# Layer 1 of a fused attention and two-layer kernel on one core: sums of y in runs of 64, their place at a tile's edge, and three pairs by the plain product

## The chip, the cores and the metric

The kernel runs on one core of one Trainium2 chip. The metric is the device time of one execution in microseconds; the kernel before takes 1069.08 us (median of 3 runs, 1069.08 to 1069.72). Lower is better.

## The reference

q, k and v are 6016 x 256. Columns of q and k are normalised, a 256 x 256 softmax matrix is built from them, and v is multiplied by it. The result goes through two layers of the same form, x @ w_in (256 x 2048), an activation, @ w_out (2048 x 256). All is float32.

```python
def _attn_ref(q, k, v, tau):
    qn = q / (np.linalg.norm(q, axis=1, keepdims=True) + 1e-06)
    kn = k / (np.linalg.norm(k, axis=1, keepdims=True) + 1e-06)
    s = kn.transpose(0, 2, 1) @ qn / tau
    a = np.exp(s - s.max(-1, keepdims=True)); a /= a.sum(-1, keepdims=True) + 1e-09
    return v @ a
# layer 1 (moe):  h = x @ w_in;  g = where(h > 0, h, exp(min(h, 0)) - 1)   (ELU);   y = g @ w_out
# layer 2 (moe2): h = y @ w_in2; g = h / (1 + exp(-h))                     (SiLU);  out = g @ w_out2
```

## The kernel before

Every float32 operand of a big product is split into a high part (an fp32r copy, written by ScalarE) and a low part (what is left, written by VectorE); a product is three matmuls, high x high, high x low, low x high (PARTS).

Four stages follow each other: the softmax matrix (to about 45 us), its product with w_in (so that layer 1 works on v itself, to about 59 us), layer 1 (to about 595 us), layer 2. Layer 1 goes through 12 tiles of columns (512 columns each, the last two 448; `ONE`, a `Phase` each), layer 2 through 6 pairs of such tiles (`TWO`). The hidden 2048 units are 16 blocks of 128, worked on as 8 pairs. So a tile has 8 slots, k = 0 to 7, written out in `slot_one` of each engine; nothing but this order and the semaphores sets the times.

In slot k of a tile the engines do this:

- TensorE (PE): `up` for the two blocks of pair k (12 matmuls), then `one_down` for pair k - 2 (LAG_PAIRS). `up` of pair k waits for VectorE's `one_g` of pair k - 2, whose banks it overwrites (`u_g`); `one_down` waits for the low parts of its pair (`u_lo`).
- ScalarE (ACT): for each block `relu` (L744) and `exp` (L749), and between them the high part of the pair before (`normal_hi` L759; for a seven-product pair `one_plain_hi` L765 and L766, `one_sums_hi` L770), which waits for that pair's `one_g`.
- VectorE (DVE): `one_g` of pair k - 1 (L1015: ELU from ScalarE's exp and the banks; waits for the second exp), then that pair's low parts (`one_pair_parts`: `normal_lo` L1020, or for a seven-product pair `one_sums` L1031 to L1036, `one_plain_lo` L1043 and L1044, `one_sums_lo` L1049).

A pair goes down in one of two ways. `normal_down` is 12 matmuls of n columns. `wino_down` is a form of Strassen's product with seven products (21 matmuls of n/2 columns) that needs the extra sums above and leaves its results in other banks, from which `y_sums` and `y_rows` make y. `Phase.wino` says which pairs go that way: none in tile 0, pairs 0, 2, 4 in tiles 1 to 8, pairs 0, 2, 4, 6 in tiles 9 to 11.

At the tile's edge come: `one_copy` (ScalarE L778, COPY_LAG = 3 slots after the last seven-product pair), `y_sums` (VectorE L1067, L1069, L1071, SUM_LAG = 4 slots after it, which is slot 0 of the next tile, or slot 2 after tiles 9 and 10), `y_rows` (VectorE L1084 twice, slot 2 of the next tile, adds the banks of the normal pairs), `y1_hi_of` (ScalarE L791 twice, slot 3) and `y1_lo_of` (VectorE L1090 twice, slot 4), which write y's two parts for layer 2 in an order in which each run takes every fourth column. In slot 4 VectorE also turns v for the tile after (L939), in slot 6 it writes its low part (L945). In tiles 1 to 8 VectorE makes the forms of w_out2 (`form_sums` slot 0, `form_lo` slot 6). In tile 0 there is instead one piece of weights in each of slots 1 to 7: `weights_hi` (ScalarE L408) at the end of the slot, `weights_lo` (VectorE L414) at the end of the same slot. SyncE loads the pieces of w_in2 two at a time: the third waits for the low part of the first.

Layer 2's first tile (`TWO[0]`) begins while the last two pairs of layer 1 go down; its first `up` waits for the last exp of layer 1.

Of the kernel before, what the change touches and what calls it, by code (L numbers as in the profile page):

```python
# [34 lines left out]
F32 = mybir.dt.float32  # L35
# [4 lines left out]
P = 128  # L40
# [22 lines left out]
M7, M5, M6, M4, M1, M2, M3 = range(N_PRODUCTS)  # L63
ONE_PRODUCTS = (M1, M5, M7, M6, M2, M3, M4)
FIRST_OF_BANK = (M1, M7, M2, M4)
WINO_FEW, WINO_MORE = (0, 2, 4), (0, 2, 4, 6)
Y_U2, Y_U4, Y_P1, Y_U5, Y_U3, Y_P5 = range(6)
Y_SUMS = 5

# [16 lines left out]
def build(nc, q, k, v, tau, w_in1, w_out1, w_in2, w_out2, out):  # L86
# [19 lines left out]
    with ctx:  # L106
# [184 lines left out]
        class Phase:  # L291
# [3 lines left out]
            def __init__(self, tile, n, before):  # L295
                self.tile, self.n, self.before = tile, n, before
                self.x = xT[tile % 2]
                self.wino = () if tile == 0 else WINO_FEW if tile in FORM_PHASES else WINO_MORE
                self.wino_before = before.wino_before + len(before.wino) if before else 0
                self.v_next = None  # L300
                if tile != NT - 1:
                    self.v_next = (tile + 1, T_LAST if tile + 1 >= NT - 2 else T, xT[1 - tile % 2])
# [58 lines left out]

        def y_raw(ph, c):

            if ph.tile == 0:
                return y_banks[c][:, 0:ph.n]
            first = (Y_U4, Y_U5)[c] * ph.n // 2
            return ysum[:, first:first + ph.n]

        pair = lambda u, k: u.number * PAIRS + k

# [119 lines left out]
        def _(sp):  # L490
# [115 lines left out]
                        x_load(0, 0, a)  # L606


            sp.wait_ge(p1_down, NT * PAIRS - 1)
            ring_load(0, 0)  # L610
            ring_load(0, 1)
            sp.wait_ge(p1_down, NT * PAIRS)
# [54 lines left out]
        def _(act):  # L667
# [105 lines left out]
            def one_copy(ph):  # L773

                act.wait_ge(p1_down, one_pair(ph, ph.wino[-1]) + 1)
                if ph.tile >= 2:
                    act.wait_ge(y1_lo, CB * ph.tile)
                act.activation(y_sum(ph, slice(Y_P1, Y_P5 + 1, Y_P5 - Y_P1)),  # L778
                               bank[4][:, 0:ph.n].rearrange("p (s x) -> p s x", s=2), ACT.Copy).then_inc(m1_copy, 1)

            def y1_hi_of(ph):


                if ph.tile == 0:
                    act.wait_ge(w_split, n_split(IN2 + N_PIECES - 1))
                    act.wait_ge(p1_down, PAIRS)
                else:
                    act.wait_ge(d_spill, 16 * ph.tile)
                    act.wait_ge(c1_sum, Y_SUMS * ph.tile)
                for c in range(CB):  # L790
                    act.activation(y1T[:, 0, c, 0:ph.n].rearrange("p (m b) -> p m b", m=4),  # L791
                                   turned_back(y_raw(ph, c), 4), ACT.Copy).then_inc(y1_hi, 1)

            def one_forms_hi():
                act.wait_ge(f1_sum, 4)
# [82 lines left out]
            def tile(u):  # L878
                for k in range(PAIRS):
                    back = shifted(u, k, 1, PAIRS)  # L880
                    if u is TWO[0] and k == 0:
                        normal_hi(ONE[-1], PAIRS - 1)
                    if u is TWO[0] and k == 1:
                        one_copy(ONE[-1])
                    for i in range(4):
                        silu_first = u is TWO[0] and k == LAG_PAIRS
                        if silu_first:
                            silu(u, k, i)
                        if back:
# [26 lines left out]
        def _(dve):  # L916
# [143 lines left out]
            def y_sums(ph):  # L1060


                n = Y_SUMS * (ph.tile - 1)
                half = lambda b, i: bank[b][:, i * ph.n // 2:(i + 1) * ph.n // 2]
                dve.wait_ge(m1_copy, ph.tile)
                dve.wait_ge(p1_down, one_pair(ph, ph.wino[-1]) + 1)
                dve.tensor_tensor(y_sum(ph, Y_U2), half(*one_m[M6]), y_sum(ph, Y_P1), ALU.add).then_inc(c1_sum, 1)  # L1067
                dve.wait_ge(c1_sum, n + 1)
                dve.tensor_tensor(y_sum(ph, Y_U3), half(*one_m[M7]), y_sum(ph, Y_U2), ALU.add).then_inc(c1_sum, 1)  # L1069
                dve.wait_ge(c1_sum, n + 2)  # L1070
                dve.tensor_tensor(y_sum(ph, slice(Y_U4, Y_U5 + 1, 2)), y_sum(ph, slice(Y_U2, Y_U3 + 1, Y_U3 - Y_U2)),  # L1071
                                  y_sum(ph, slice(Y_P5, Y_P5 + 1)).broadcast_to([P, 2, ph.n // 2]),
                                  ALU.add).then_inc(c1_sum, 1)

            def y_rows(ph):

                n = Y_SUMS * (ph.tile - 1)
                dve.wait_ge(c1_sum, n + 3)
                for c in range(CB):
                    if c == 0:  # L1080
                        dve.wait_ge(y_done, ph.tile + 1)
                    else:
                        dve.wait_ge(p1_down, one_pair(ph, PAIRS - 1) + 1)
                    dve.tensor_tensor(y_raw(ph, c), y_banks[c][:, 0:ph.n], y_raw(ph, c), ALU.add).then_inc(c1_sum, 1)  # L1084

            def y1_lo_of(ph):
                for c in range(CB):
                    dve.wait_ge(y1_hi, CB * ph.tile + c + 1)
                    hi, lo = (y1T[:, x, c, 0:ph.n].rearrange("p (m b) -> p m b", m=4) for x in range(2))
                    dve.tensor_tensor(lo, turned_back(y_raw(ph, c), 4), hi.bitcast(F32),  # L1090
                                      ALU.subtract).then_inc(y1_lo, 1)

            def one_forms_sums():

# [44 lines left out]
            def slot_one(ph, k):  # L1139
                back = shifted(ph, k, 1, PAIRS)  # L1140
                if ph.tile == 1 and k == SLOT_ROWS:
                    y1_lo_of(ONE[0])
                if back:
                    one_g(*back)
                for tile in (ph, ph.before):
                    if tile and tile.wino and k + PAIRS * (tile is not ph) == tile.wino[-1] + SUM_LAG:
                        y_sums(tile)
                if ph.tile > 1 and k == SLOT_ROWS:
                    y_rows(ph.before)
                if back:  # L1150
                    one_pair_parts(*back)
                if ph.tile > 1 and k == SLOT_Y1_LO:
                    y1_lo_of(ph.before)
                if k == SLOT_V_TURN and ph.v_next:
                    v_transpose(*ph.v_next[:2])
                if k == SLOT_V_LO and ph.v_next:
                    vT_lo(*ph.v_next)
                if weights_in_slot(ph, k) is not None:
                    weights_lo(dve, weights_in_slot(ph, k))
                if ph.tile == 0 and k == SLOT_ONE_FORMS_SUM:  # L1160
                    one_forms_sums()
                if ph.tile == 0 and k == SLOT_ONE_FORMS_LO:
# [83 lines left out]
            def tile(u):  # L1246
                for k in range(PAIRS):
                    back = shifted(u, k, 1, PAIRS)
                    if u is TWO[0] and k == 0:
                        one_g(ONE[-1], PAIRS - 1)  # L1250
                        one_pair_parts(ONE[-1], PAIRS - 1)
                    if u is TWO[0] and k == 1:
                        y_sums(ONE[-1])
                    if back:
                        pair_sums(*back, 2)
# [52 lines left out]
        def _(pe):  # L1308
# [99 lines left out]
                elif ph.tile:  # L1408
                    pe.wait_ge(c1_sum, Y_SUMS * (ph.tile - 2) + 4 + c)

            def normal_down(ph, k):
                pe.wait_ge(u_lo, 2 * one_pair(ph, k) + 2)
                if k == 0:
                    pe.wait_ge(p_lo, CB * NWC)
                if ph.tile == 0:
                    pe.wait_ge(w_split, n_split(OUT1 + (2 * k + 1) * C // WP))
                for c in range(CB):
                    for n, (i, (x, y)) in enumerate((i, xy) for i in range(2) for xy in PARTS):
                        weights = wout1[:, 2 * k + i, x, c * P:(c + 1) * P]
                        g = by_turns(gpn[k % 2][:, y, i, 0:ph.n])  # L1420
                        last = k == PAIRS - 1 and n == 5
                        if ph.wino and k == 1 and c == 1 and n == 0:

                            for h in range(2):
                                pe.matmul(y_banks[c][:, h * ph.n // 2:(h + 1) * ph.n // 2], weights,
                                          g[:, h * ph.n // 4:(h + 1) * ph.n // 4, :], start=False, stop=False)
                        else:
                            mm = pe.matmul(y_banks[c][:, 0:ph.n], weights, g, start=k == 0 and n == 0, stop=last)  # L1428
                    if c == 0 and k == PAIRS - 1:
                        mm.then_inc(y_done, 1)  # L1430
                mm.then_inc(p1_down, 1)

            def wino_down(ph, k, first=0, end=N_PRODUCTS * len(PARTS)):

# [34 lines left out]
            def pair_up(u, k, i):  # L1469
# [7 lines left out]
                if u is TWO[0] and k < LAG_PAIRS:  # L1477
                    if k == 0 and i % 2 == 0:
                        pe.wait_ge(u_g, NT * PAIRS - 1 + i // 2)

                    pe.wait_ge(u_act, up_of(u, 0, 0) + H_FREE[4 * k + i])
                else:
                    pe.wait_ge(u_act, up_of(u, k, i))
                product(h_bank(u, k, i)[:, 0:u.n],
# [34 lines left out]
            def tile(u):  # L1519
                for k in range(PAIRS):  # L1520
                    back = shifted(u, k, LAG_PAIRS, PAIRS)
                    for i in range(4):
# [51 lines left out]
```

## Time and profile before

| | before |
|---|---|
| median of 3 runs | 1069.08 us (1069.08 to 1069.72) |
| the profiled execution | 1070.87 us |
| its span, first to last instruction | 1069.1 us |
| TensorE busy | 1023.8 us, 96% of the span |
| VectorE busy | 831.3 us, 78% |
| ScalarE busy | 722.0 us, 68% |
| mean granted TensorE clock | 0.986 |

Busy times are for the whole span, and matmuls are pipelined, so that a busy TensorE can still be fed late. What one step of the change is worth is read from the stage in which it lies.

### The profile page before, as it was taken

How to read it: one execution, taken by the hardware profiler on the slowest of the kernel's cores; microseconds unless marked ns; L12 is line 12 of the kernel's file. 1: busy time of each engine (PE TensorE's matmuls, PEld its weight loads, DVE VectorE, ACT ScalarE, POOL GpSimd, SP SyncE). 2: the span in 40 equal slices, each digit the busy share in tenths (PEclk: the TensorE clock that was granted, in tenths of full speed). 3: DMA queues.
4: the chain of work that ended last, by engine and by line, in shares of the span. 5: the costliest groups of instructions: out<-in, count | busy, mean ns of one | idle time of the engine just before them, and what ended most of it. 6: DMA issues, size and time to landing. Idle time of an engine off the chain costs nothing.

```text
span 1069.1 us, 14152 instructions
## 1 busy us (share of the span) xinstructions
PE 1023.8 (96%) x5085; PEld 904.8 (85%) x5085; DVE 831.3 (78%) x963; ACT 722.0 (68%) x1097; POOL 10.2 (1%) x11
## 2 busy tenths in 40 slices
PE   9997999999999899998999999999999999999998
PEld 8876787888888788887899878888888888888997
DVE  7767788878888787887878677787787787787786
ACT  6676667778667776777777665666666655666664
POOL 0300000000000000000000000000000000000000
PEclk9998999999999999999999999999999999999999
DMA  9902021221302213022030316425424434435333
GB/s 349 346 5 69 40 65 47 58 59 45 104 30 74 60 45 104 1 91 57 1 119 35 130 43 248 154 101 143 181 74 140 181 103 111 169 103 141 106 89 89
DMA packets 115066, 109.83 MB, mean 103 GB/s; under 512 B 89024, under 2 KB 97216, under 8 KB 112448
## 3 DMA queue, kind: packets, MB, share of 16 engines
q1 hardware_dynamic: 114400, 108.58, 31.7%
q8 instruction: 35, 0.57, 0.2%
q10 hardware_dynamic: 608, 0.49, 0.1%
q14 instruction: 23, 0.19, 0.1%
HBM read 83.23 MB, written 25.82 MB: 102 GB/s over the span
## 4 chain that ended last, share of the span: by engine, by line
PE 42%; DVE 23%; ACT 15%; issue 9%; DVEq 0%; ACTq 0%
PE banks L1314 22%; PE banks L1511 19%; ACT g_raw L749 6%; DVE g_raw L1015 5%; ACT g_raw L744 3%; DVE g_parts L1020 3%; ACT y1T_parts L791 2%; DVE g_raw_forms L1031 2%; ACT g_parts L759 2%; DVE y1T_parts L1090 2%; DVE g_form_parts L1043 2%; DVE g_raw_forms L1034 1%; DVE g_raw_forms L1036 1%; DVE v_transposed L939 1%; DVE g_form_parts L1044 1%
## 5 line engine op out<-in xcount | busy, mean ns | idle before, releaser
L1314 PE MATMUL banks<-xT_parts,a_w_in 128*128 128x512 f32 (+1 forms) x1152 | 271.3, 387 | 23.3 <-DVE g_raw L1015 23.2
L1314 PE MATMUL banks<-x_parts,w_in_parts 128*128 128x512 f32 (+1 forms) x1152 | 276.4, 376 | 4.7 <-ACT g_pair L850 2.6
L1314 PEld LDWEIGHTS banks<-xT_parts,a_w_in 128*128 128x128 f32 x1152 | 220.3, 195 | 56.9 <-DVE g_raw L1015 26.4
L1314 PEld LDWEIGHTS banks<-x_parts,w_in_parts 128*128 128x128 f32 x1152 | 215.9, 190 | 34.6 <-ACT g_pair L850 4.5
L1511 PE MATMUL banks<-g_pair_parts,w_forms 128*128 128x512 f32 (+1 forms) x987 | 239.3, 375 | 0.0
L1511 PEld LDWEIGHTS banks<-g_pair_parts,w_forms 128*128 128x128 f32 x987 | 186.5, 189 | 22.1
L850 ACT ACTIVATE g_pair<-banks 128x512 f32<-128x512 f32 (+1 forms) x192 | 112.9, 588 | 134.6 <-PE banks L1314 127.8
L1428 PE MATMUL banks<-g_parts,w_out_parts 128*128 128x512 f32 (+1 forms) x709 | 162.6, 376 | 0.0
L1428 PEld LDWEIGHTS banks<-g_parts,w_out_parts 128*128 128x128 f32 x709 | 133.7, 190 | 16.3
L1015 DVE SCALAR_TENSOR_TENSOR g_raw<-g_raw,banks 128x1024 f32<-128x1024 f32 (+1 forms) x96 | 114.5, 1193 | 25.0 <-ACT g_raw L749 25.0
L1197 DVE TENSOR_TENSOR g_pair_parts<-g_forms,g_pair_parts 128x1024 fp32r<-128x1024 f32 (+1 forms) x96 | 115.2, 1201 | 21.9 <-ACT g_pair_parts L859 21.8
L1020 DVE TENSOR_TENSOR g_parts<-g_raw,g_parts 128x1024 fp32r<-128x1024 f32 (+1 forms) x60 | 72.4, 1207 | 69.1 <-ACT g_parts L759 68.6
L859 ACT ACTIVATE g_pair_parts<-g_forms 128x1024 fp32r<-128x1024 f32 (+1 forms) x96 | 99.4, 1037 | 37.1 <-PE banks L1511 33.2
L749 ACT ACTIVATE g_raw<-g_raw 128x512 f32<-128x512 f32 (+1 forms) x192 | 118.1, 615 | 3.1
L744 ACT ACTIVATE g_raw<-banks 128x512 f32<-128x512 f32 (+1 forms) x192 | 110.0, 573 | 1.3 <-PE banks L1314 1.3
L1184 DVE TENSOR_TENSOR g_forms<-g_pair 128x1024 f32<-128x1024 f32 (+1 forms) x48 | 57.7, 1202 | 65.7 <-ACT g_pair L850 65.6
L759 ACT ACTIVATE g_parts<-g_raw 128x1024 fp32r<-128x1024 f32 (+1 forms) x60 | 62.6, 1043 | 56.0 <-issue 47.8
L1203 DVE TENSOR_TENSOR g_pair_parts<-g_pair,g_pair_parts 128x1536 fp32r<-128x1536 f32 (+1 forms) x48 | 82.5, 1719 | 3.5 <-ACT g_pair_parts L866 3.5
L866 ACT ACTIVATE g_pair_parts<-g_pair 128x1024 fp32r<-128x1024 f32 (+1 forms) x96 | 78.8, 822 | 0.6 <-PE banks L1511 0.6
L765 ACT ACTIVATE g_form_parts<-g_raw 128x512 fp32r<-128x512 f32 (+1 forms) x36 | 22.4, 622 | 78.5 <-DVE g_raw L1015 78.5
L1452 PE MATMUL banks<-g_form_parts,w_out_parts 128*128 128x256 f32 (+1 forms) x324 | 56.9, 285 | 10.7 <-DVE g_form_parts L1049 5.6
L1452 PEld LDWEIGHTS banks<-g_form_parts,w_out_parts 128*128 128x128 f32 x324 | 47.5, 195 | 19.0 <-DVE g_form_parts L1049 10.3
(112 smaller groups left out, 855.2 us busy)
## 6 DMA issues: line engine op xcount, KB each, us to landing
w_forms<-w_forms SPq DMA_DIRECT2D x48, 896.0 KB, 4.7
y_parts<-y1T_parts SPq DMA_DIRECT2D x10, 1024.0 KB, 4.1
x_parts<-y_parts SPq DMA_DIRECT2D x10, 1024.0 KB, 7.0
w_forms<-w_out_forms SPq DMA_DIRECT2D x8, 896.0 KB, 4.2
early_qk<-q SPq DMA_DIRECT2D x23, 256.0 KB, 7.7
early_qk<-k SPq DMA_DIRECT2D x22, 256.0 KB, 8.0
out<-out_tile SPq DMA_DIRECT2D x40, 128.0 KB, 2.7
v_in<-v SPq DMA_DIRECT2D x36, 128.0 KB, 3.6
```

Source lines behind the costliest of these rows:

```text
L744: act.activation(raw_units(ph, k)[:, i, :], h_ps[f % 4][:, 0:ph.n], ACT.Relu, scale=-1.0).then_inc(u_relu, 1)
L749: act.activation(e, e, ACT.Exp, scale=-1.0).then_inc(u_act, 1)
L759: act.activation(gpn[k % 2][:, 0, :, 0:ph.n], raw_units(ph, k), ACT.Copy).then_inc(u_hi, 2)
L850: act.activation(g2[:, k % 2, i, 0:u.n], h_bank(u, k, i)[:, 0:u.n], ACT.Silu).then_inc(u_act, 1)
L859: act.activation(gp2[k % 2][:, 0, 3 + 2 * s:5 + 2 * s, 0:u.n], t_sb[:, 2 * s:2 * s + 2, 0:u.n], ACT.Copy).then_inc(t_hi, 1)
L1015: dve.scalar_tensor_tensor(g, g, -1.0, two_banks[k % 2][:, :, 0:ph.n], ALU.add, ALU.max).then_inc(u_g, 1)
L1020: dve.tensor_tensor(part(1), raw_units(ph, k), part(0).bitcast(F32), ALU.subtract).then_inc(u_lo, 2)
L1197: dve.tensor_tensor(part(1), t_sb[:, 2 * s:2 * s + 2, 0:u.n], part(0).bitcast(F32), ALU.subtract).then_inc(t_lo, 1)
L1314: mm = pe.matmul(dst, lhsT, rhs, start=first and n == 0, stop=last and n == len(todo) - 1)
L1428: mm = pe.matmul(y_banks[c][:, 0:ph.n], weights, g, start=k == 0 and n == 0, stop=last)
L1452: mm = pe.matmul(bank[b][:, half * ph.n // 2:(half + 1) * ph.n // 2], weights, by_turns(gpw[:, y, operand, 0:ph.n // 2]), start=k == 0 and ...
L1511: mm = pe.matmul(m_banks[m][:, 0:u.n], ring[k % N_RING][:, form, x, :], by_turns(gp2[k % 2][:, y, operand, 0:u.n]), start=k == 0 and part ...
```

## The change

- `y_sum`'s slots hold each half of a tile as four runs of 64 (of 56 in a short tile) in place of plain order. The reading by every fourth column moves from `y1_hi_of` and `y1_lo_of`, which read SBUF, to `one_copy`, `y_sums` and `y_rows`, which read the banks.
- `Phase.wino` is (0, 2, 4) in every tile but tile 0. So pair 6 of tiles 9, 10, 11 is a normal pair; `one_copy` of these tiles comes in slot 7, `y_sums` in slot 0 of what follows.
- VectorE's slot: `y_rows` comes ahead of `one_g`; `y_sums` comes behind `one_pair_parts`.
- `weights_lo` of a piece comes one slot after its `weights_hi`.
- At the layer boundary the first four `up` of layer 2 no longer wait for the last exp of layer 1; a normal pair goes down in four shares between them; SyncE's wait ahead of the first two loads of the ring is for an earlier pair.

```diff
-WINO_FEW, WINO_MORE = (0, 2, 4), (0, 2, 4, 6)
+ONE_WINO = (0, 2, 4)
-                self.wino = () if tile == 0 else WINO_FEW if tile in FORM_PHASES else WINO_MORE
+                self.wino = ONE_WINO if tile else ()
         def y_raw(ph, c):
-            if ph.tile == 0:
-                return y_banks[c][:, 0:ph.n]
             first = (Y_U4, Y_U5)[c] * ph.n // 2
-            return ysum[:, first:first + ph.n]
+            return ysum[:, first:first + ph.n].rearrange("p (h m b) -> p h m b", h=2, m=4)
+        half_turned = lambda x: x.rearrange("p (b m) -> p m b", m=4)
+        half_plain = lambda x: x.rearrange("p (m b) -> p m b", m=4)
+        def y_and_part(ph, c, x):
+            part = y1T[:, x, c, 0:ph.n]
             if ph.tile == 0:
+                return turned_back(y_banks[c][:, 0:ph.n], 4), part.rearrange("p (m b) -> p m b", m=4)
+            return y_raw(ph, c).rearrange("p h m b -> p m h b"), part.rearrange("p (m h b) -> p m h b", m=4, h=2)
...
-            sp.wait_ge(p1_down, NT * PAIRS - 1)
+            sp.wait_ge(p1_down, one_pair(ONE[-1], ONE[-1].wino[-1]) + 1)
...
-                dve.tensor_tensor(y_sum(ph, Y_U2), half(*one_m[M6]), y_sum(ph, Y_P1), ALU.add).then_inc(c1_sum, 1)
+                dve.tensor_tensor(half_plain(y_sum(ph, Y_U2)), half_turned(half(*one_m[M6])),
+                                  half_plain(y_sum(ph, Y_P1)), ALU.add).then_inc(c1_sum, 1)
...
-                    dve.tensor_tensor(y_raw(ph, c), y_banks[c][:, 0:ph.n], y_raw(ph, c), ALU.add).then_inc(c1_sum, 1)
+                    dve.tensor_tensor(y_raw(ph, c), y_banks[c][:, 0:ph.n].rearrange("p (h b m) -> p h m b", h=2, m=4),
+                                      y_raw(ph, c), ALU.add).then_inc(c1_sum, 1)
...
             def slot_one(ph, k):          # VectorE
                 back = shifted(ph, k, 1, PAIRS)
+                if ph.tile > 1 and k == SLOT_ROWS:
+                    y_rows(ph.before)
                 if back:
                     one_g(*back)
+                    one_pair_parts(*back)
                 for tile in (ph, ph.before):
                     if tile and tile.wino and k + PAIRS * (tile is not ph) == tile.wino[-1] + SUM_LAG:
                         y_sums(tile)
-                if ph.tile > 1 and k == SLOT_ROWS:
-                    y_rows(ph.before)
-                if back:
-                    one_pair_parts(*back)
...
-                if weights_in_slot(ph, k) is not None:
-                    weights_lo(dve, weights_in_slot(ph, k))
+                if back and weights_in_slot(*back) is not None:
+                    weights_lo(dve, weights_in_slot(*back))
...
-                    pe.wait_ge(u_act, up_of(u, 0, 0) + H_FREE[4 * k + i])
+                if u is TWO[0] and k < LAG_PAIRS:
+                    if H_FREE[4 * k + i]:
+                        pe.wait_ge(u_act, up_of(u, 0, 0) + H_FREE[4 * k + i])
...
                         elif k == 0:
-                            wino_down(ONE[-1], PAIRS - 2, *PARTS_OF_SLOT[i:i + 2])
+                            normal_down(ONE[-1], PAIRS - 2, 3 * i, 3 * i + 3)
```

## Rows read from the trace of the kernel before

**Rows 1.** Waits of PE over the span: us in total, times, longest.

```profile
PE banks L1314 <- DVE g_raw L1015: 23.2, 14, 4.2
```

**Rows 2.** Stretches: length, busy (count) of PE, PEld, DVE, ACT, POOL, clock, DMA.

```profile
300.00:345.00 45.00, 41.60 (x221) 36.27 (x220) 36.57 (x48) 33.09 (x54) 0.00 (x0) 1.00 0.22 62
...
650.00:1053.00 403.00, 403.00 (x1908) 358.33 (x1907) 316.67 (x314) 250.54 (x354) 0.00 (x0) 1.00 0.42 132
```

**Rows 3.** PE in order of time, tile 4: start, length, line, idle before.

```profile
320.35 2.86 PE L1314 MATMUL banks<-xT_parts,a_w_in 128*128 128x512 f32 x12 [1.90 <-DVE g_raw L1015]
...
324.35 0.60 PE L1452 MATMUL banks<-g_form_parts,w_out_parts 128*128 128x256 f32 x3 [1.14 <-DVE g_form_parts L1049]
```

**Rows 4.** DVE in order of time, slot 4 of tile 4 to slot 2 of tile 5.

```profile
309.73 1.22 DVE L1015 SCALAR_TENSOR_TENSOR g_raw<-g_raw,banks 128x1024 f32<-128x1024 f32 x1 [0.44 <-ACT g_raw L749]
313.92 1.23 DVE L1020 TENSOR_TENSOR g_parts<-g_raw,g_parts 128x1024 fp32r<-128x1024 f32 x1 [2.97 <-ACT g_parts L759]
315.06 2.98 DVE L1090 TENSOR_TENSOR y1T_parts<-y_sums,y1T_parts 128x512 fp32r<-128x512 f32 x2
...
319.13 1.17 DVE L1015 SCALAR_TENSOR_TENSOR g_raw<-g_raw,banks 128x1024 f32<-128x1024 f32 x1
...
324.73 1.22 DVE L1015 SCALAR_TENSOR_TENSOR g_raw<-g_raw,banks 128x1024 f32<-128x1024 f32 x1 [0.44 <-ACT g_raw L749]
...
330.76 1.22 DVE L1015 SCALAR_TENSOR_TENSOR g_raw<-g_raw,banks 128x1024 f32<-128x1024 f32 x1
333.22 1.22 DVE L1020 TENSOR_TENSOR g_parts<-g_raw,g_parts 128x1024 fp32r<-128x1024 f32 x1 [1.25 <-ACT g_parts L759]
334.81 1.22 DVE L1015 SCALAR_TENSOR_TENSOR g_raw<-g_raw,banks 128x1024 f32<-128x1024 f32 x1 [0.37 <-ACT g_raw L749]
...
337.48 1.22 DVE L1020 TENSOR_TENSOR g_parts<-g_raw,g_parts 128x1024 fp32r<-128x1024 f32 x1
...
339.55 1.21 DVE L1015 SCALAR_TENSOR_TENSOR g_raw<-g_raw,banks 128x1024 f32<-128x1024 f32 x1
...
343.53 1.22 DVE L1049 TENSOR_TENSOR g_form_parts<-g_raw_forms,g_form_parts 128x1024 fp32r<-128x1024 f32 x1 [0.19 <-ACT g_form_parts L770]
345.20 1.22 DVE L1015 SCALAR_TENSOR_TENSOR g_raw<-g_raw,banks 128x1024 f32<-128x1024 f32 x1 [0.45 <-ACT g_raw L749]
346.34 1.28 DVE L1084 TENSOR_TENSOR y_sums<-banks,y_sums 128x512 f32<-128x512 f32 x2
```

**Rows 5.** ACT in order of time, from the end of slot 3 of tile 4.

```profile
309.60 2.78 ACT L791 ACTIVATE y1T_parts<-y_sums 128x512 fp32r<-128x512 f32 x2
```

**Rows 6.** Groups by line, shapes kept apart: busy us, mean ns, idle before.

```profile
L1090 DVE TENSOR_TENSOR y1T_parts<-y_sums,y1T_parts 128x512 fp32r<-128x512 f32 x18 | 25.9, 1481 | 0.0
...
L1090 DVE TENSOR_TENSOR y1T_parts<-banks,y1T_parts 128x512 fp32r<-128x512 f32 x2 | 1.3, 687 | 0.9 <-ACT y1T_parts L791 0.9
...
L945 DVE TENSOR_TENSOR xT_parts<-v_transposed,xT_parts 128x512 fp32r<-128x512 f32 x18 | 11.6, 684 | 0.0
...
L671 ACT ACTIVATE xT_parts<-v_transposed 128x512 fp32r<-128x512 f32 x18 | 10.2, 618 | 0.0
```

**Rows 7.** DVE in order of time, tile 0.

```profile
62.97 1.22 DVE L1015 SCALAR_TENSOR_TENSOR g_raw<-g_raw,banks 128x1024 f32<-128x1024 f32 x1 [2.41 <-ACT g_raw L749]
...
80.28 1.22 DVE L414 TENSOR_TENSOR w_out_parts<-early_w_out,w_out_parts 128x1024 fp32r<-128x1024 f32 x1 [1.31 <-ACT w_out_parts L408]
...
93.61 1.23 DVE L414 TENSOR_TENSOR w_in_parts<-weight_stage,w_in_parts 128x1024 fp32r<-128x1024 f32 x1 [2.35 <-ACT w_in_parts L408]
...
111.84 1.22 DVE L1015 SCALAR_TENSOR_TENSOR g_raw<-g_raw,banks 128x1024 f32<-128x1024 f32 x1
```

**Rows 8.** PE at the start of layer 2.

```profile
595.24 1.92 PE L1314 MATMUL banks<-x_parts,w_in_parts 128*128 128x512 f32 x6 [2.10 <-ACT g_raw L749]
...
611.96 0.81 PE L1511 MATMUL banks<-g_pair_parts,w_forms 128*128 128x512 f32 x3
...
626.72 1.56 PE L1314 MATMUL banks<-x_parts,w_in_parts 128*128 128x512 f32 x6 [1.65 <-ACT g_pair L850]
```

More of the change, by code:

```diff
@@ L362, in y_raw @@
         def y_raw(ph, c):
+            first = (Y_U4, Y_U5)[c] * ph.n // 2
+            return ysum[:, first:first + ph.n].rearrange("p (h m b) -> p h m b", h=2, m=4)
[3 more added lines that the diff above has]
+            part = y1T[:, x, c, 0:ph.n]
             if ph.tile == 0:
-                return y_banks[c][:, 0:ph.n]
-            first = (Y_U4, Y_U5)[c] * ph.n // 2
-            return ysum[:, first:first + ph.n]
+                return turned_back(y_banks[c][:, 0:ph.n], 4), part.rearrange("p (m b) -> p m b", m=4)
+            return y_raw(ph, c).rearrange("p h m b -> p m h b"), part.rearrange("p (m h b) -> p m h b", m=4, h=2)
         pair = lambda u, k: u.number * PAIRS + k
@@ L777, in one_copy @@
                     act.wait_ge(y1_lo, CB * ph.tile)
-                act.activation(y_sum(ph, slice(Y_P1, Y_P5 + 1, Y_P5 - Y_P1)),
-                               bank[4][:, 0:ph.n].rearrange("p (s x) -> p s x", s=2), ACT.Copy).then_inc(m1_copy, 1)
+                act.activation(y_sum(ph, slice(Y_P1, Y_P5 + 1, Y_P5 - Y_P1)).rearrange("p s (m b) -> p s m b", m=4),
+                               bank[4][:, 0:ph.n].rearrange("p (s b m) -> p s m b", s=2, m=4), ACT.Copy).then_inc(m1_copy, 1)
             def y1_hi_of(ph):
@@ L790, in y1_hi_of @@
                 for c in range(CB):
-                    act.activation(y1T[:, 0, c, 0:ph.n].rearrange("p (m b) -> p m b", m=4),
-                                   turned_back(y_raw(ph, c), 4), ACT.Copy).then_inc(y1_hi, 1)
+                    y, part = y_and_part(ph, c, 0)
+                    act.activation(part, y, ACT.Copy).then_inc(y1_hi, 1)
             def one_forms_hi():
@@ L882, in tile @@
                         normal_hi(ONE[-1], PAIRS - 1)
-                    if u is TWO[0] and k == 1:
-                        one_copy(ONE[-1])
                     for i in range(4):
@@ L1066, in y_sums @@
                 dve.wait_ge(p1_down, one_pair(ph, ph.wino[-1]) + 1)
-                dve.tensor_tensor(y_sum(ph, Y_U2), half(*one_m[M6]), y_sum(ph, Y_P1), ALU.add).then_inc(c1_sum, 1)
+                dve.tensor_tensor(half_plain(y_sum(ph, Y_U2)), half_turned(half(*one_m[M6])),
+                                  half_plain(y_sum(ph, Y_P1)), ALU.add).then_inc(c1_sum, 1)
                 dve.wait_ge(c1_sum, n + 1)
-                dve.tensor_tensor(y_sum(ph, Y_U3), half(*one_m[M7]), y_sum(ph, Y_U2), ALU.add).then_inc(c1_sum, 1)
+                dve.tensor_tensor(half_plain(y_sum(ph, Y_U3)), half_turned(half(*one_m[M7])),
+                                  half_plain(y_sum(ph, Y_U2)), ALU.add).then_inc(c1_sum, 1)
                 dve.wait_ge(c1_sum, n + 2)
@@ L1088, in y1_lo_of @@
                     dve.wait_ge(y1_hi, CB * ph.tile + c + 1)
-                    hi, lo = (y1T[:, x, c, 0:ph.n].rearrange("p (m b) -> p m b", m=4) for x in range(2))
-                    dve.tensor_tensor(lo, turned_back(y_raw(ph, c), 4), hi.bitcast(F32),
-                                      ALU.subtract).then_inc(y1_lo, 1)
+                    (y, hi), (_, lo) = (y_and_part(ph, c, x) for x in range(2))
+                    dve.tensor_tensor(lo, y, hi.bitcast(F32), ALU.subtract).then_inc(y1_lo, 1)
             def one_forms_sums():
@@ L1251, in tile @@
                         one_pair_parts(ONE[-1], PAIRS - 1)
-                    if u is TWO[0] and k == 1:
                         y_sums(ONE[-1])
@@ L1409, in rows_free, with normal_down @@
                     pe.wait_ge(c1_sum, Y_SUMS * (ph.tile - 2) + 4 + c)
-            def normal_down(ph, k):
-                pe.wait_ge(u_lo, 2 * one_pair(ph, k) + 2)
+            def normal_down(ph, k, first=0, end=2 * 2 * len(PARTS)):
+                if first == 0:
+                    pe.wait_ge(u_lo, 2 * one_pair(ph, k) + 2)
                 if k == 0:
@@ L1416, in normal_down @@
                     pe.wait_ge(w_split, n_split(OUT1 + (2 * k + 1) * C // WP))
[L1417 to L1429, printed above, removed]
+                for n in range(first, end):
+                    c, i, (x, y) = n // 6, n // 3 % 2, PARTS[n % 3]
+                    weights = wout1[:, 2 * k + i, x, c * P:(c + 1) * P]
+                    g = by_turns(gpn[k % 2][:, y, i, 0:ph.n])
+                    if ph.wino and k == 1 and n == 6:
+                        for h in range(2):
+                            pe.matmul(y_banks[c][:, h * ph.n // 2:(h + 1) * ph.n // 2], weights,
+                                      g[:, h * ph.n // 4:(h + 1) * ph.n // 4, :], start=False, stop=False)
+                    else:
+                        mm = pe.matmul(y_banks[c][:, 0:ph.n], weights, g, start=k == 0 and n % 6 == 0,
+                                       stop=k == PAIRS - 1 and n % 6 == 5)
+                    if n == 5 and k == PAIRS - 1:
                         mm.then_inc(y_done, 1)
-                mm.then_inc(p1_down, 1)
+                    if n == 11:
+                        mm.then_inc(p1_down, 1)
             def wino_down(ph, k, first=0, end=N_PRODUCTS * len(PARTS)):
```

## The prediction

> **What bounds the kernel now.** First the waits of PE: of the 45 us of the span in which it was not busy, 23.2 us went, in 14 waits of up to 4.2 us, to the ELU of layer 1 (`one_g`, L1015) [rows 1]. Then the stretches: layer 2, from 650 to 1053 us, has PE busy for all of its 403.00 us, so nothing that happens there can be hidden or regained and every microsecond won ahead of it reaches the end; a tile of layer 1 has PE busy for 41.60 of 45.00 us [rows 2]. Last the timeline of one tile. PE waits 1.90 us for an ELU and 1.14 us for low parts [rows 3], both on VectorE. The ELU of the same slot starts at 319.13, and PE's matmuls at 320.35 [rows 3, 4]. So layer 1 is not bound by PE. It is bound by a chain that goes to and fro between VectorE and ScalarE: ELU, its high part, the next exps, the next ELU. The reader is to read the starts of L1015 in rows 4 as the beat of that chain: 309.73, 319.13, 324.73, 330.76, 334.81, 339.55, 345.20, steps of 9.40, 5.60, 6.03, 4.05, 4.74 and 5.65 us. With the 4.07 us and the 5.66 us of slots 2 and 3, worked from the same timeline, they make a tile of 45.2 us. PE's own work in it is the floor: at most 41.8 us by its busy share [rows 2], and 40.8 by its matmuls, which follow each other at about 0.21 us per 512 columns (403.00 us over 1908 [rows 2]; closer, by the timeline, 16 `up` at 1.30, five normal pairs at 2.59, three of seven products at 2.34).
>
> **The change, part by part.**
>
> 1. *The order of y's sums.* Writing y's high part takes 2.78 us for two halves [rows 5], its low part 2.98 us [rows 4], 1481 ns each over 18 of them, against 684 ns (VectorE) and 618 ns (ScalarE) for the same 512 columns read from SBUF in runs of 32 [rows 6]. With runs of 64 I take these two values: ScalarE wins 1.6 us per tile and VectorE 1.6 us. Both lie on the chain, one behind the other: in that slot VectorE sits idle for 2.97 us until ScalarE, delayed by L791, has written the high part (313.92), then writes y's low part, turns v and only then comes to the ELU [rows 4]. Step 9.40 becomes 6.2 or less: -3.2 us. Is the reading by fours dear in its new place? The row nearest to it is y's low part of tile 0, which reads the banks by every fourth column and an SBUF operand: 687 ns [rows 6]; I take no cost. The other end is the SBUF price: 0.8 us more per 512 columns, in `y_rows` twice and in `y_sums` once, 2.4 us a tile on the chain.
>
> 2. *`y_sums` behind the low parts.* Now it fills the time in which VectorE waits for the high part: in the slot without it that gap is 1.25 us (333.22, 2.46 us after its ELU), in the slot with it L1020 follows at once (337.48, 2.67 us after) [rows 4]. It took 1.53 us (334.81 + 1.14 to 337.48). In the new order: 2.46 us to the low part, 1.14 for it (313.92 to 315.06), 1.53 for `y_sums`, 0.93 for the sums of w_out2's forms, 6.06 us in all instead of 4.74: +1.3 us. Behind the waiting low part `y_sums` itself now queues; PE needs it only in slot 2.
>
> 3. *`y_rows` ahead of the ELU.* The low parts of the pair before leave VectorE free at 343.53 + 1.14 = 344.67; the exps are ready at 345.20. Two `y_rows` take 1.2 us, to 345.87: the ELU is 0.7 us late [rows 4]. Its own wait, for the last normal pair, is over by then, as PE works two slots ahead of it. What it wins, some 0.4 us of PE in that slot, is off the chain.
>
>    Parts 1 to 3 on tiles 2 to 8: -3.2 + 1.3 + 0.7 = -1.2, and by the single rows of this tile (y's writes 1.65 instead of 1.6 us each) -1.3 us. Seven tiles: **-9 us**. A tile is then 43.9 us, still over PE's 40.8; PE is next late for the low parts of pairs 0 and 4, as now.
>
> 4. *Three pairs by the plain product.* The chain's step with a seven-product pair is 5.65 us (339.55 to 345.20), with a normal one 4.05 [rows 4]: -1.6 us for tile 9, 1.4 for each short one (x 448/512). PE gets 0.25 us more in tile 9 and nothing in the short ones; it has that room. With it `y_sums` comes away from slot 2, where it stood between two ELUs in tiles 10 and 11 (-1 us each) and goes to slot 0. Tile 9: -3.2 (y), -1.6, +1.1 (part 2 without forms), +0.7: -3.1. Tiles 10 and 11: -2.7 each, the same at 7/8. Together **-8.5 us**.
>
> 5. *`weights_lo` a slot later*, tile 0. Its ELUs go from 62.97 to 111.84 [rows 7] in seven steps, of 6.15 us but for two (9.71 and 8.41), since VectorE waits for the high part of the same slot's piece: 1.31 us in an ordinary slot, 2.35 us in the one in which ScalarE writes v's first [rows 7]. A slot later the piece is ready: steps of 2.46 + 1.14 + 1.14 = 4.74. Slot 1 (no piece any more) wins 2.1, slots 2 and 3 1.4 each, slot 4 0.25 (it turns v in that gap), slot 5 2.4, slot 6 0.2, slot 7 1.4: 9.2 us, less 1.14 for the last piece in slot 0 of tile 1. **-8 us**. PE (5.2 us a slot) keeps up but for short waits. On SyncE's queue the loads of the third and fourth piece of w_in2 go out a slot later relative to the work, and the load of the first forms behind them; these took 4.0 us to land in this stretch, and ScalarE wants them 6.3 and about 4 us after. The last has no room; it costs up to 0.5 us of ScalarE, beside the chain.
>
> 6. *The layer boundary.* PE idles 2.10 us until the last exp, and then runs at a granted clock of 0.90 over the next stretch: 16.72 us from 595.24 to 611.96 [rows 8] for matmuls that take 14.9 at full rate (8 `up` at 1.30, 24 of 448 columns at 0.189). Without the wait and the gap: -0.6 and -1.8. PE then waits 1.65 us for a SiLU [rows 8] that is behind y's high part on ScalarE (2.6 us there), and 0.75 us for one behind the low part; with these at half, -2.2. **-4.6 us**. The earlier ring loads win nothing; they had landed.
>
> Sum: -9 - 8.5 - 8 - 4.6 = -30 us. The profiled execution took 1070.87 us, 1.8 over its span and 1.8 over the median of 1069.08, so that it comes to 1040.7 and the median to **1039 us**.
>
> By the skill: the row shows 1481 ns for a reading of SBUF by every fourth float and 684 ns for runs [rows 6]. The Trainium skill (SBUF — State Buffer, the section on ports, its note on "cachelines") says that SBUF has lines of 16 bytes and that each access that crosses to a new line pays; the trace agrees. The same note gives PSUM lines of 8 bytes and a slowdown of matmuls for any non-contiguous access, which speaks against moving the stride there; for VectorE's reading the 687 ns row does not agree, and for a matmul's no run here shows it.
>
> **Rivals.**
>
> A. *The stride costs in the banks what it cost in SBUF.* 2.4 us on the chain for ten tiles: -30 + 24 = 1063 us. For it: the new instructions have a walk of four dimensions that no row has. Against: 687 ns. 8%. (This is what the PSUM rule named above would do here if it held for VectorE.)
>
> B. *y's writes are slow for another reason than the stride*, such as meeting PE's and the other engine's reads at that moment, and stay at 1.4 us. For it: the same two instructions took only 1.05 us each in tile 10, by its timeline. Then parts 2 and 3 stand alone: +2.0 us on seven tiles, +14, tiles 9 to 11 -2, boundary -2.4, tile 0 -8: +2 us, 1071; and with the loads of part 5 late, up to 1079. This is the slower case, and it decides from where a write of y keeps over 1.2 us. Against: tile 0's 687 ns. 6%.
>
> C. *PE becomes the bound again.* Its slack falls to 3 us a tile, in gaps of up to 1.4 us; where the granted clock falls to 1.2 GHz, as it did after 4.2 us of waiting in tile 0, a slot of 5.2 us takes up to 3 us more. If half of the ten tiles lose 2 us: 1049 us, range 1044 to 1056. 17%.
>
> D. *The change takes the chain below what I counted*, as gaps close that I left: 1031 us. 4%.
>
> **How the numbers follow.** The forecast, 1039 (1034 to 1044), has 65%; A 8, B 6, C 17, D 4. To hold 8 in 10 the range takes forecast and C: 1033 to 1056. A measurement of this kernel tells 0.2%, 2.1 us, from no change. Faster: all but B, less 0.01 for what I have not thought of, 0.93; B divided, 0.03 within and, with that 0.01, 0.04 slower.
>
> **What would show it.** L1090 and L791 on y_sums near 690 and 620 ns; L1084 and L1067 as before (683, 418); steps of L1015 at an edge of 6.1 and 6.3 us and of 6.1 in place of 9.4; ELUs of tile 0 ending near 103; layer 2's first matmul near 569; a tile of 43.9 us. Wrong: a tile of 45 us or more, L1084 over 1 us, or PE idle in layer 2's steady part.

## The result, and the profile after

The changed kernel takes 1039.74 us (median of 4 runs, 1038.93 to 1039.96) against 1069.08: ratio 0.9724, 95% interval 0.9707 to 0.9741. The forecast was 1039. The profiled execution took 1039.91 us, its span is 1038.1, 31.0 us less than before; VectorE is busy for 806.8 us and ScalarE for 702.1, some 25 and 20 less; the mean granted TensorE clock is 1.0.

One slip of names first: the stretch that the rows and the prediction call tiles 4 and 5 holds, counted from 0 as the kernel counts, tiles 5 and 6. No number depends on it.

The waits of PE in the kernel after, where [rows 1] stood, and the two stretches that answer to [rows 2] (columns as there):

```profile
PE banks L1460 <- DVE g_form_parts L1055: 17.1, 17, 1.1
PE banks L1320 <- DVE g_raw L1021: 2.8, 4, 1.5
```

```profile
285.00:328.00 43.00, 41.03 (x218) 35.42 (x217) 34.04 (x49) 31.59 (x54) 0.00 (x0) 1.00 0.23 64
625.00:1020.00 395.00, 395.00 (x1869) 351.13 (x1868) 311.12 (x309) 246.29 (x347) 0.00 (x0) 1.00 0.41 129
```

The waits for the ELU have gone from 23.2 to 2.8 us, and what is next late is what the prediction named, the low parts of seven-product pairs: 17.1 us in 17 waits, two in each of tiles 2 to 8 and one in tiles 1, 9 and 10. PE still does not bind layer 1, and layer 2 still has no idle time.

VectorE of the kernel after over one edge, for [rows 4]; L1021 is the ELU, L1026 the low part of a normal pair, L1099 y's low part, L1073 the first of `y_sums`, L1092 `y_rows`:

```profile
300.12 1.22 DVE L1021 SCALAR_TENSOR_TENSOR g_raw<-g_raw,banks 128x1024 f32<-128x1024 f32 x1 [0.44 <-ACT g_raw L757]
302.66 1.23 DVE L1026 TENSOR_TENSOR g_parts<-g_raw,g_parts 128x1024 fp32r<-128x1024 f32 x1 [1.32 <-ACT g_parts L767]
303.80 1.29 DVE L1099 TENSOR_TENSOR y1T_parts<-y_sums,y1T_parts 128x512 fp32r<-128x512 f32 x2
...
306.17 1.18 DVE L1021 SCALAR_TENSOR_TENSOR g_raw<-g_raw,banks 128x1024 f32<-128x1024 f32 x1
...
321.86 1.22 DVE L1021 SCALAR_TENSOR_TENSOR g_raw<-g_raw,banks 128x1024 f32<-128x1024 f32 x1 [0.36 <-ACT g_raw L757]
324.33 1.23 DVE L1026 TENSOR_TENSOR g_parts<-g_raw,g_parts 128x1024 fp32r<-128x1024 f32 x1 [1.24 <-ACT g_parts L767]
325.47 0.42 DVE L1073 TENSOR_TENSOR y_sums<-banks,y_sums 128x256 f32<-128x256 f32 x1
...
327.92 1.22 DVE L1021 SCALAR_TENSOR_TENSOR g_raw<-g_raw,banks 128x1024 f32<-128x1024 f32 x1
...
331.92 1.23 DVE L1055 TENSOR_TENSOR g_form_parts<-g_raw_forms,g_form_parts 128x1024 fp32r<-128x1024 f32 x1 [0.20 <-ACT g_form_parts L778]
333.06 1.28 DVE L1092 TENSOR_TENSOR y_sums<-banks,y_sums 128x512 f32<-128x512 f32 x2
334.26 1.21 DVE L1021 SCALAR_TENSOR_TENSOR g_raw<-g_raw,banks 128x1024 f32<-128x1024 f32 x1
```

The reader is to see three steps from ELU to ELU. 300.12 to 306.17 is 6.05 us where it was 9.40: the wait ahead of the low part is 1.32 us instead of 2.97, and y's low part takes 1.29 instead of 2.98. 321.86 to 327.92 is 6.06 where it was 4.74: VectorE idles 1.24 us ahead of L1026, and `y_sums` comes only behind it. 327.92 to 334.26 is 6.34 where it was 5.65: `y_rows` stands in front of an ELU that could have begun.

The groups that answer to [rows 6]:

```profile
L1099 DVE TENSOR_TENSOR y1T_parts<-y_sums,y1T_parts 128x512 fp32r<-128x512 f32 x18 | 11.6, 684 | 0.0
...
L1092 DVE TENSOR_TENSOR y_sums<-banks,y_sums 128x512 f32<-128x512 f32 x18 | 11.5, 682 | 0.0
...
L800 ACT ACTIVATE y1T_parts<-y_sums 128x512 fp32r<-128x512 f32 x18 | 10.2, 615 | 0.0
```

y's two writes are at the price of runs, and `y_rows`, which now reads the banks by fours, is as before (682 ns; it was 683 by the same view of before).

VectorE in tile 0, for [rows 7]; the last ELU of tile 0 comes at 103.34 us instead of 111.84, and no weight piece (L422) has a wait in front of it:

```profile
63.71 1.22 DVE L1021 SCALAR_TENSOR_TENSOR g_raw<-g_raw,banks 128x1024 f32<-128x1024 f32 x1 [2.42 <-ACT g_raw L757]
...
71.39 1.22 DVE L422 TENSOR_TENSOR w_out_parts<-early_w_out,w_out_parts 128x1024 fp32r<-128x1024 f32 x1
...
103.34 1.21 DVE L1021 SCALAR_TENSOR_TENSOR g_raw<-g_raw,banks 128x1024 f32<-128x1024 f32 x1
```

PE at the start of layer 2, for [rows 8]; from 568.68 to 583.58 are 14.90 us, which were 16.72, and the wait for the SiLU behind y's high part is no longer shown:

```profile
568.68 1.46 PE L1320 MATMUL banks<-x_parts,w_in_parts 128*128 128x512 f32 x6
...
583.58 0.81 PE L1520 MATMUL banks<-g_pair_parts,w_forms 128*128 128x512 f32 x3
...
596.79 1.56 PE L1320 MATMUL banks<-x_parts,w_in_parts 128*128 128x512 f32 x6
```

Where the 31.0 us came from, by the starts of the ELU in both timelines and the rows above. The edge from tile 8 to tile 9 (+1.07 us) is counted with the tiles behind it, as in the forecast. The first line is no effect of the change: in the ten profiled executions of this case the first ELU starts between 62.8 and 64.2 us.

| stretch | before | after | difference | forecast |
|---|---|---|---|---|
| start to the first ELU | 62.97 | 63.71 | +0.7 | 0 |
| to the first ELU of tile 1 | 53.40 | 45.30 | -8.1 | -8 |
| to the first ELU of tile 9, without the edge's +1.07 | 358.31 | 348.69 | -9.6 | -9 |
| that edge, and to the last ELU of layer 1 | 120.45 | 111.64 | -8.8 | -8.5 |
| to the first matmul of a layer 2 pair going down | 16.83 | 14.24 | -2.6 | -2.4 |
| to the end | 457.14 | 454.52 | -2.6 | -2.2 |

### The profile page after: what moved, and what is told of

Read it like the earlier page. It is cut to its first block, busy times and chain, and to the rows that moved or that the text cites. A ratio compares the mean times of both kernels' runs of the same rounds, so it can differ in the third digit from the quotient of the medians.

```text
span 1038.1 us, 14074 instructions
## 1 busy us (share of the span) xinstructions
PE 1011.3 (97%) x5058; PEld 893.4 (86%) x5058; DVE 806.8 (78%) x948; ACT 702.1 (68%) x1091; POOL 10.2 (1%) x11
## 4 chain that ended last, share of the span: by engine, by line
PE 49%; DVE 18%; ACT 12%; issue 9%; DVEq 0%; ACTq 0%
PE banks L1320 25%; PE banks L1520 20%; DVE g_raw L1021 4%; ACT g_raw L757 4%; ACT g_raw L752 3%; ACT g_parts L767 3%; PE banks L1434 2%; DVE g_parts L1026 2%; DVE g_raw_forms L1037 2%; DVE g_raw_forms L1040 1%; DVE g_raw_forms L1042 1%; PE banks L1460 1%; ACT g_form_parts L778 1%; DVE g_form_parts L1049 1%; DVE v_transposed L945 1%
## 5 line engine op out<-in xcount | busy, mean ns | idle before, releaser
L1320 PE MATMUL banks<-xT_parts,a_w_in 128*128 128x512 f32 (+1 forms) x1152 | 261.1, 376 | 2.9 <-DVE g_raw L1021 2.8
L1320 PEld LDWEIGHTS banks<-xT_parts,a_w_in 128*128 128x128 f32 x1152 | 213.5, 189 | 33.2 <-DVE g_raw L1021 5.3
L1434 PE MATMUL banks<-g_parts,w_out_parts 128*128 128x512 f32 (+1 forms) x745 | 170.4, 375 | 0.0
L1434 PEld LDWEIGHTS banks<-g_parts,w_out_parts 128*128 128x128 f32 x745 | 139.9, 189 | 16.7 <-DVE g_parts L1026 0.3
L1026 DVE TENSOR_TENSOR g_parts<-g_raw,g_parts 128x1024 fp32r<-128x1024 f32 (+1 forms) x63 | 75.9, 1204 | 79.0 <-ACT g_parts L767 79.0
L1021 DVE SCALAR_TENSOR_TENSOR g_raw<-g_raw,banks 128x1024 f32<-128x1024 f32 (+1 forms) x96 | 114.4, 1191 | 20.7 <-ACT g_raw L757 20.7
L767 ACT ACTIVATE g_parts<-g_raw 128x1024 fp32r<-128x1024 f32 (+1 forms) x63 | 65.3, 1037 | 56.3 <-issue 54.0
L1460 PE MATMUL banks<-g_form_parts,w_out_parts 128*128 128x256 f32 (+1 forms) x297 | 52.2, 285 | 17.9 <-DVE g_form_parts L1055 17.1
L1460 PEld LDWEIGHTS banks<-g_form_parts,w_out_parts 128*128 128x128 f32 x297 | 41.3, 191 | 29.1 <-DVE g_form_parts L1055 28.2
```

Source lines behind the costliest of these rows:

```text
L767: act.activation(gpn[k % 2][:, 0, :, 0:ph.n], raw_units(ph, k), ACT.Copy).then_inc(u_hi, 2)
L1021: dve.scalar_tensor_tensor(g, g, -1.0, two_banks[k % 2][:, :, 0:ph.n], ALU.add, ALU.max).then_inc(u_g, 1)
L1026: dve.tensor_tensor(part(1), raw_units(ph, k), part(0).bitcast(F32), ALU.subtract).then_inc(u_lo, 2)
L1320: mm = pe.matmul(dst, lhsT, rhs, start=first and n == 0, stop=last and n == len(todo) - 1)
L1460: mm = pe.matmul(bank[b][:, half * ph.n // 2:(half + 1) * ph.n // 2], weights, by_turns(gpw[:, y, operand, 0:ph.n // 2]), start=k == 0 and ...
```

## The experiments

**1. runs_only**: the order of y's sums alone, on the kernel before.

```diff
+            return ysum[:, first:first + ph.n].rearrange("p (h m b) -> p h m b", h=2, m=4)
...     (with y_and_part, and one_copy, y_sums, y_rows, y1_lo_of as in the change; all else as before)
```

> The kernel before with the sums of y in runs of 64 and nothing else of the change. Theory (the chain between VectorE and ScalarE is the bound, and steps add up): the step of 9.4 us goes to 6.05, the others stay, a tile is 41.9 us; -3.3 us on eight tiles, -1.85 and -1.6 on the short ones, -2.2 at the boundary: -32 us, 1037 us, more than the whole change gave. Rival (PE takes over as soon as the chain is shorter, so the steps do not add up): a tile stays at 43 us or more, PE's waits only move, 1047 us or more.

Measured: 1036.42 us (1036.35 to 1037.42), ratio 0.9691, interval 0.9675 to 0.9707. The step of a middle tile is 6.05 us, the others are those of before, a tile is 41.85 us. So the steps add up as the chain says, and the first part by itself is worth more (-33 us) than the whole change.

**2. sums_in_gap** and **3. both_back**: the two orders at the edge, taken back one after the other.

```diff
 # sums_in_gap, against the change
                 if back:
                     one_g(*back)
-                    one_pair_parts(*back)
                 for tile in (ph, ph.before):
                     if tile and tile.wino and k + PAIRS * (tile is not ph) == tile.wino[-1] + SUM_LAG:
                         y_sums(tile)
+                if back:
+                    one_pair_parts(*back)
```

```diff
 # both_back: y_rows stands here too, behind y_sums, and no longer ahead of one_g
+                if ph.tile > 1 and k == SLOT_ROWS:
+                    y_rows(ph.before)
                 if back:
                     one_pair_parts(*back)
```

> The changed kernel with y_sums put back between the ELU and the low parts; y_rows stays ahead of the ELU. Theory (chain): the step into an edge goes from 6.06 back to 4.73 us on seven tiles, 5.13 to about 4.05, 3.9 and 3.7 on the last three: -12.6 us, 1027 us. Rival (y_sums was rightly moved: PE and ScalarE gain from the earlier low parts, or PE is the bound by now): 1039 us or more.

> The changed kernel with y_sums and y_rows both back between ELU and low parts, all else of the change kept. Theory (chain): a tile is 41.9 us, PE's work of 40.8 still fits with 0.65 us of waiting for y_rows in slot 2; -2.0 us on seven tiles, -1.7, -1.9 and -1.5 on the last three: -19 us, 1021 us. Rival (PE's wait for y_rows in slot 2 was worth the move): +0.4 us on ten tiles, 1044 us.

Measured: 1028.19 us (1027.05 to 1028.26; ratio 0.9608, interval 0.9592 to 0.9624) and 1022.60 us (1022.13 to 1023.17; ratio 0.9557, interval 0.9541 to 0.9573). The steps into an edge are 4.72 us in both, and the one at `y_rows` 6.33 in the first and 5.65 in the second. Both moves of the change therefore cost time: 11.6 us and 5.6 us. What `y_rows` ahead of the ELU buys can be seen in the waits of PE in both_back, of which these are the two largest (the next is 1.4 us, for low parts):

```profile
PE banks L1461 <- DVE y_sums L1092: 3.1, 7, 0.6
PE banks L1321 <- DVE g_raw L1021: 2.8, 4, 1.5
```

3.1 us of PE for `y_rows`, in a kernel in which PE has that time. The times came 1.2 and 1.6 us above the expectation, as PE, at 40.8 of 41.86 us, is now nearly level with the chain. In both kernels the first matmul of layer 2 starts 0.3 us behind the last ELU, where in the change it started 0.7 us ahead of it, and PE is busy for all of tile 11 (32.00 of 32.00 us in the one, 33.60 of 33.60 in the other). In tile 11 of both_back two steps are also longer than in the change (4.71 us where it was 4.35, and 4.35 where it was 3.67).

**4. weights_same_slot**: `weights_lo` back in the slot of its `weights_hi`, all else of the change kept.

```diff
-                if back and weights_in_slot(*back) is not None:
-                    weights_lo(dve, weights_in_slot(*back))
+                if weights_in_slot(ph, k) is not None:
+                    weights_lo(dve, weights_in_slot(ph, k))
```

> The changed kernel with weights_lo back in the slot of its weights_hi. Theory (chain): tile 0 takes 8.0 us longer to its last ELU and the first of tile 1, and nothing of it is regained: 1047.7 us. Rival (PE, which waits in tile 1 for low parts anyway, takes most of it back): under 1043 us.

Measured: 1047.29 us (1047.03 to 1047.83), 7.6 us over the change, ratio to before 0.9789 (0.9772 to 0.9805). The steps of tile 0 are again 6.15 us but for two. Nothing of the loss is regained later: from the first ELU to the end the profiled execution takes 982.6 us against 974.4.

**5. plain_pairs_only**: three normal pairs, on the kernel before.

```diff
-                self.wino = () if tile == 0 else WINO_FEW if tile in FORM_PHASES else WINO_MORE
+                self.wino = ONE_WINO if tile else ()
...
-                            wino_down(ONE[-1], PAIRS - 2, *PARTS_OF_SLOT[i:i + 2])
+                            normal_down(ONE[-1], PAIRS - 2, 3 * i, 3 * i + 3)
```

> The kernel before with the normal product for pair 6 of tiles 9 to 11 (and what hangs on it: one_copy in slot 7, y_sums in slot 0 of the tile after, the four shares at the boundary) and nothing else; y_sums stands in the gap between ELU and low parts. Theory (chain): -1.6 us in tile 9, -1.2, -0.45 and -1.5 in tile 10, -0.9 and -1.5 in tile 11: -7 us, 1062 us, though PE gets more columns. Rival (PE is what counts, and it gets 0.9 us more at full rate): 1070 us.

Measured: 1062.13 us (1061.49 to 1062.49), ratio 0.9934 (0.9919 to 0.9950). The step behind pair 6 is 4.06 us (5.65) and 3.65 us (5.12). These three steps give 4.5 us. The rest comes from `y_sums`, which no longer stands between two ELUs: the steps of slot 2 in tiles 10 and 11 fall from 4.85 and 4.58 to 3.66 us. So the product with more multiplications is faster here, because it asks for fewer sums of the two engines that bind.

**6. last_exp_wait**: the change with the wait for the last exp of layer 1.

```diff
-                    if H_FREE[4 * k + i]:
-                        pe.wait_ge(u_act, up_of(u, 0, 0) + H_FREE[4 * k + i])
+                    pe.wait_ge(u_act, up_of(u, 0, 0) + H_FREE[4 * k + i])
```

> The changed kernel with the first ups of layer 2 again waiting for the last exp of layer 1. Theory: PE comes 0.7 us later (569.3 instead of 568.7) and nothing else: 1040.4 us, hardly to be told from the change. Rival (it is this wait that made PE idle and lowered its clock): +2.4 us or more, 1042 us.

Measured: 1039.57 us (1039.21 to 1040.45); the medians show no difference from the change. The profiled executions do: from the first ELU to the end it takes 975.2 us with the wait and 974.4 without, 0.8 us, where the theory said 0.7. PE waits once more, 0.60 us, and over the next 15 us its granted clock is 1.00, that is 2.4 GHz:

```profile
568.98 1.53 PE L1320 MATMUL banks<-x_parts,w_in_parts 128*128 128x512 f32 x6 [0.60 <-ACT g_raw L757]
```

So the wait as such was worth 0.8 us. The rest of what the boundary gave came from the shorter chain ahead of it: `runs_only` and `plain_pairs_only` keep the wait as well, and there too the gap is 0.70 and 0.64 us instead of 2.10 and the granted clock behind it 1.00 instead of 0.90.

**7. gap_fill**: both_back, and more side work between an ELU and the low parts of a normal pair.

```diff
                 if back:
                     one_g(*back)
...     (y_sums, y_rows as in both_back)
+                if k == SLOT_V_TURN and ph.v_next:
+                    v_transpose(*ph.v_next[:2])
+                if k == SLOT_V_LO and ph.v_next:
+                    vT_lo(*ph.v_next)
+                if back and weights_in_slot(*back) is not None:
+                    weights_lo(dve, weights_in_slot(*back))
                 if back:
                     one_pair_parts(*back)
...     (the same three are taken out behind y1_lo_of)
```

> both_back, and also the turning of v (slot 4), v's low part (slot 6) and the weights' low parts (tile 0) moved from behind the low parts of a normal pair into the 1.25 us in which VectorE waits for their high part. Theory (chain until PE's work is reached): the chain would be 39.5 us a tile, PE's 40.8 binds; -0.9 us on eight tiles and about -3 in tile 0: 1012 to 1015 us, with PE waiting for nothing in the middle tiles and ScalarE's relu waiting for PE instead. Rival (the gap is not free: work there delays the low parts, for which PE waits): 1022 us or more.

Measured: 1008.55 us (1008.06 to 1008.89), ratio 0.9433 (0.9419 to 0.9448), the fastest of all, 31 us faster than the change and 3.5 below the lower end of the expectation. A middle tile takes 40.71 us, against the 40.8 that the prediction gave as PE's floor. Slot 4 of one, VectorE, and a stretch of 40 us:

```profile
280.50 1.22 DVE L1021 SCALAR_TENSOR_TENSOR g_raw<-g_raw,banks 128x1024 f32<-128x1024 f32 x1 [0.44 <-ACT g_raw L757]
281.64 1.24 DVE L945 STREAM_TRANSPOSE v_transposed<-v_in 128x1024 f32<-128x1024 f32 x1
283.36 1.22 DVE L1026 TENSOR_TENSOR g_parts<-g_raw,g_parts 128x1024 fp32r<-128x1024 f32 x1 [0.49 <-ACT g_parts L767]
```

```profile
265.00:305.00 40.00, 40.00 (x219) 35.92 (x218) 34.31 (x47) 31.69 (x54) 0.00 (x0) 1.00 0.25 69
```

The turning of v (L945) now lies in the wait, of which 0.49 us are left, PE is busy for 40.00 of 40.00 us, and the wait has changed sides: ScalarE's relu waits for PE.

```profile
ACT g_raw L752 <- PE banks L1321: 37.2, 39, 1.6
```

In both_back that wait was 4.5 us. PE is the bound of the middle tiles at last. The surplus over the expectation lies in two places. Up to the first ELU of tile 1 it takes 40.1 us, where both_back took 45.3 and I had counted on -3; tiles 1 to 8 are 10.8 us shorter than in both_back, where I had counted on 7.2, the most in tiles 1 and 2 (1.9 and 2.0 us). Against it, tiles 9 to 11 are 1.8 us longer.

**8. plain_order_reads**: a question about the old cost of y's writes, on the kernel before.

```diff
-        by_turns = lambda x: x.rearrange("p (a b) -> p b a", a=2)
+        by_turns = lambda x: x.rearrange("p (b a) -> p b a", a=2)
```

> The kernel before with the moving operand of every matmul read in plain order, where it was read in turns from the two halves of a tile (1024 bytes apart at 512 columns); the columns come out in another order, so the results are not the reference's, the amount of work is the same. It asks why y's writes, which read every fourth column, took 1.52 us beside 512-column tiles and 1.10 us in tile 10 beside 448-column ones. If it is the meeting with PE's reads in turns: L1090 falls to 1.1 us or below in all tiles and the time to about 1060 us. If it is not: L1090 stays at 1.5 us beside 512-column tiles.

Measured, in a single run: 1084.61 us; its results are not the reference's, as its columns come out in another order. The first half came true, the time did not. The group of y's low part in it, and a stretch of its layer 2 beside one of before:

```profile
L1090 DVE TENSOR_TENSOR y1T_parts<-y_sums,y1T_parts 128x512 fp32r<-128x512 f32 x18 | 18.5, 1067 | 0.0
```

```profile
700.00:1060.00 360.00, 360.00 (x1602) 301.10 (x1601) 272.68 (x270) 210.43 (x297) 0.00 (x0) 1.00 0.39 119
```

```profile
700.00:1050.00 350.00, 350.00 (x1660) 311.72 (x1659) 279.99 (x278) 217.83 (x308) 0.00 (x0) 1.00 0.41 127
```

A reading of SBUF by every fourth float takes 1.07 us beside these matmuls, not 1.48; the rest was the meeting with PE's reads in turns. The kernel before shows the same by itself. Its y's low parts of 448 columns stand once beside matmuls of 448 columns (first row) and once beside those of 512, at the start of layer 2 (second row), 979 and 1380 ns each; with reads in plain order both are at 969 ns.

```profile
579.44 1.88 DVE L1090 TENSOR_TENSOR y1T_parts<-y_sums,y1T_parts 128x448 fp32r<-128x448 f32 x2
...
634.86 2.68 DVE L1090 TENSOR_TENSOR y1T_parts<-y_sums,y1T_parts 128x448 fp32r<-128x448 f32 x2
```

The step of 9.40 us fell to 7.79. But PE needs 0.225 us per matmul (360 / 1602) where it needed 0.211 (350 / 1660), and it binds layer 2, so that the whole is 15 us slower.

## Why the prediction was right

*The bound.* That the chain VectorE, ScalarE, VectorE sets layer 1, and not PE, held in the change and in experiments 1 to 6, but for tile 11 of experiments 2 and 3: times followed from the sum of its steps, to within 2 us of the whole, also where PE's work grew (experiment 5). It ended where the prediction put PE's floor (experiment 7).

*Part 1.* Forecast 1.6 us for each engine and 3.2 together; measured 3.35 (9.40 to 6.05). The slightly larger gain comes from this tile's writes having been above the mean. Taking 684 and 618 ns from instructions that read in runs of 32 was the right row: 684 and 615. The banks read by fours cost nothing, as the one row of it had said (687 ns).

*Parts 2 and 3.* Forecast +1.3 and +0.7 us a tile, measured +1.32 and +0.69. They were losses by the chain's arithmetic, and experiments 2 and 3 show them as such.

*Part 4.* Forecast -8.5 for tiles 9 to 11, measured -8.8 (the terms written down for tile 9 give -3.0, not -3.1). The plain product and the place of `y_sums` alone, on the kernel before, gave 6.8 us, 7 expected.

*Part 5.* Forecast steps of 4.74 us, measured 4.75 and 4.73; -8 against -8.1. The late load cost 0.4 us of ScalarE in one wait for a piece of w_in2, beside the chain, as forecast (up to 0.5).

*Part 6.* Forecast -4.6, measured -5.2, and in part by luck. The prediction put -2.4 down to the removed wait and the gap. The wait is worth 0.8 us (experiment 6); the clock came back in every kernel with a shorter chain ahead of the boundary, with the wait in place. So this edit was given what parts 1 and 4 bring by themselves. The -2.2 for the SiLU waits stood for waits of 2.4 us and became -2.6: 0.2 us of waiting are left, as y's two writes there take 1.04 and 1.15 us instead of 2.58 and 2.68. The four shares and SyncE's earlier wait were not run by themselves.

*The rivals.* A fell with L1092 at 682 ns. B fell with L1099 at 684 ns; yet its premise had something in it: about half of the old cost beyond 684 ns, (1481 - 1067) / (1481 - 684), was not the stride but the company, the matmuls beside it (experiment 8). It did not decide, since runs avoid both. C did not come: the granted clock is 1.0, with 17 gaps of up to 1.1 us for low parts and four of up to 1.5 for the ELU. D did not come in the change, as it leaves its two losses in place.

The Trainium skill (SBUF — State Buffer, the note on "cachelines" in the section on the DMA port swizzle) says that each access that crosses to a new 16-byte line of SBUF pays a penalty. The runs agree: VectorE took 1067 ns where its pattern changes line with every float, beside matmuls in plain order, against 684 in runs. The note's rule for PSUM is about matmuls, and no run here tests it.

## What to carry to other kernels

Before an instruction is moved, look for what bounds the stage, and write down that chain's steps with their waits; here the steps that the edits change could each be priced to 0.2 us in this way, and two of the edits were losses hidden in a sum of gains. Side work belongs into the gap in which the bounding engine waits for its partner (1.25 us in each normal pair here), not behind the wait, and not ahead of the step that the partner waits for. A product with fewer multiplications is no gain while the engines that prepare its sums bind.

## What the runs showed of the hardware that was not expected

A VectorE instruction that reads 512 columns of SBUF took 684 ns in runs of 64. By every fourth float it took 1067 ns when the matmuls beside it read their moving operand in plain order, 1100 ns beside matmuls of 448 columns read in turns (halves 896 bytes apart), and 1529 ns beside those of 512 columns in turns (halves 1024 bytes apart). So what one engine's stride costs depends on another's. And the matmul of 512 fp32r columns was faster read in turns from two halves, 0.216 us, than in plain order, 0.229 (280 us of layer 2 over 1299 and over 1221 matmuls, all of 512 columns; the 0.211 and 0.225 above have some of 448 among them). The plain order was run once. Why, stays open; a bank of SBUF that both reads meet in would fit, and was not tested.
